# Waiting for an expert's weights block by block, and a third rounding remainder moved to GpSimd

## What is computed

```
x -> attention of 512 tokens and 32 state rows per (batch, head), 8 x 8 heads        -> 4352 rows of 512
idx = argmax(logits);  h = max(x[mask] @ w1[e], 0);  out[mask] = gate * (h @ w2[e])  -> 8 experts, 512 -> 1024 -> 512
h = x @ w_in;  g = max(h, 0) + alpha * min(h, 0);  out = g @ w_out                   -> 512 -> 2048 -> 512
```

## Time and profile before

| | us |
|---|---|
| device time, median of 3 (lowest, highest) | 1403.92 (1402.19, 1405.24) |
| device time of the profiled execution | 1405.78 |
| its span, first to last instruction | 1404.0 |
| TensorE busy in it | 1343.3 (96%) |
| VectorE, ScalarE, GpSimd busy | 826.7, 424.1, 189.4 |
| mean granted TensorE clock | 0.979 of full |

### The profile page before, as it was taken

How to read it: one execution, slowest core, us unless ns; L and a number is a source line. 1 busy time by engine, 2 the same in 40 slices (tenths; PEclk the granted TensorE clock), 3 DMA queues, 4 the chain that set the end, 5 groups by cost and what they waited for, 6 DMA issues and landing times.

```text
span 1404.0 us, 22418 instructions
## 1 busy us (share of the span) xinstructions
PE 1343.3 (96%) x7807; PEld 1159.1 (83%) x7808; DVE 826.7 (59%) x1070; ACT 424.1 (30%) x623; POOL 189.4 (13%) x234
## 2 busy tenths in 40 slices
PE   8999589999979999997899999999999999999998
PEld 7877468888868888885899999999978888888886
DVE  4777653223555435255677767778876566566653
ACT  5888241111433323144112202122322222222221
POOL 4564112211222222222000000000000000000000
PEclk9999799999999999999899999999999999999999
DMA  7785263111547433451633344333444444444453
GB/s 286 266 272 187 68 217 105 37 45 63 199 157 244 149 115 128 167 161 59 212 134 120 127 143 142 128 135 111 163 121 114 120 120 128 118 112 112 112 120 53
DMA packets 180849, 195.50 MB, mean 139 GB/s; under 512 B 25296, under 2 KB 130768, under 8 KB 180176
## 3 DMA queue, kind: packets, MB, share of 16 engines
q1 hardware_dynamic: 173552, 174.61, 39.4%
q0 software_dynamic: 6112, 19.93, 4.1%
q10 hardware_dynamic: 1152, 0.56, 0.2%
HBM read 127.16 MB, written 67.37 MB: 139 GB/s over the span
## 4 chain that ended last, share of the span: by engine, by line
PE 92%; DVE 3%; ACT 2%; issue 1%; ACTq 0%; DMA 0%; DVEq 0%; POOL 0%; POOLq 0%
PE ps_p L364 13%; PE ps_p L366 13%; PE ps_p L365 13%; PE ps_y L364 5%; PE ps_y L366 5%; PE ps_y L365 5%; PE ps_h L364 5%; PE ps_h L366 5%; PE ps_h L365 5%; PE ps_o L364 5%; PE ps_o L366 5%; PE ps_o L365 5%; PE ps_hT L1514 2%; PE ps_sr L1392 1%; PE ps_xT L1508 1%
## 5 line engine op out<-in xcount | busy, mean ns | idle before, releaser
L364 PE MATMUL ps_p<-b_hi,w_hi 128*128 128x272 f32 x896 | 259.5, 290 | 3.7 <-DVE b_lo L1227 3.7
L366 PE MATMUL ps_p<-b_hi,w_lo 128*128 128x272 f32 x896 | 259.7, 290 | 0.0
L365 PE MATMUL ps_p<-b_lo,w_hi 128*128 128x272 f32 x896 | 259.6, 290 | 0.0
L364 PEld LDWEIGHTS ps_p<-b_hi,w_hi 128*128 128x128 f32 x896 | 169.8, 190 | 4.6 <-DVE b_lo L1227 4.6
L366 PEld LDWEIGHTS ps_p<-b_hi,w_lo 128*128 128x128 f32 x896 | 170.0, 190 | 0.0
L365 PEld LDWEIGHTS ps_p<-b_lo,w_hi 128*128 128x128 f32 x896 | 169.3, 189 | 0.0
L364 PE MATMUL ps_h<-w_hi,xgT_hi 128*128 128x512 f32 x296 | 122.4, 413 | 9.7 <-DVE w_lo L952 7.7
L1147 DVE COPY hid<-ps_h 128x512 f32<-128x512 f32 x74 | 51.1, 691 | 135.2 <-PE ps_h L366 128.7
L364 PE MATMUL ps_y<-w_hi,hidT_hi 128*128 128x512 f32 x296 | 122.7, 414 | 0.0
L1149 DVE SCALAR_TENSOR_TENSOR hidT_lo<-ps_hT,hidT_hi 128x512 fp32r<-128x512 f32 x74 | 51.2, 691 | 121.2 <-ACT hidT_hi L828 121.2
L828 ACT ACTIVATE hidT_hi<-ps_hT 128x512 fp32r<-128x512 f32 x74 | 44.2, 598 | 245.1 <-PE ps_hT L1514 245.1
(11 more groups left out here) (223 smaller groups left out, 2417.7 us busy)
## 6 DMA issues: line engine op xcount, KB each, us to landing
acts<-gb SPq DMA_DIRECT2D x128, 272.0 KB, 2.1
stage<-in_moe_w SPq DMA_DIRECT2D x32, 1024.0 KB, 5.2
gt<-acts SPq DMA_DIRECT2D x32, 1024.0 KB, 6.1
xs_all<-in_xT SPq DMA_DIRECT2D x8, 1024.0 KB, 6.3
xN_all<-in_xN SPq DMA_DIRECT2D x8, 1024.0 KB, 6.2
rows_x<-xrow SPq DMA_DIRECT2D x32, 256.0 KB, 2.7
out_rows<-orow SPq DMA_DIRECT2D x32, 256.0 KB, 2.0
yz<-rows_y SPq DMA_DIRECT2D x30, 256.0 KB, 3.1
```

The lines of the kernel that those rows point to most:

```text
L364: pe.matmul(out, s_hi, m_hi, start=start, stop=False)
L365: pe.matmul(out, s_hi, m_lo, start=False, stop=False)
L366: return pe.matmul(out, s_lo, m_hi, start=False, stop=stop)
```

## The change

It has four parts.

1. TensorE waits for chunk 0 at an expert's start, and in every slot for chunk 1 before the third k block of `hidden(0)`, for chunk 2 before `result(0)`, and for chunk 3 before `result(1)`. These three waits compare with a value held in a register and stand in the slot's loop, so that they are run 37 times.
2. The low part of the third late block is made by GpSimd, after its last scatter, with a semaphore of its own, `late_lo_ready`. TensorE's P3 waits for that, and VectorE waits for it before the first write over `late_w` (`low` of P7).
3. ScalarE issues its four loads of y after two late roundings and makes the third behind them.
4. A pad of 32 columns moves `late_w`, so that it lies under the low parts of P7 and later alone.

```diff
@@ memory
+        sb("late_pad", [P, 32], c=sc)
         late_w = [t[:].rearrange("p a k f -> p (a k f)") for t in (raw_w, sum_w)] + [sb("late_w", [P, CW], c=sc)[:]]
@@ gpsimd, after the loop of slots
+            pool.wait_ge(w_hi_ready, (E + 1) * CH + 3)
+            pool.tensor_tensor(w_lo[1][:, 2 * CW:3 * CW], late_w[2], w_hi[1][:, 2 * CW:3 * CW].bitcast(F32), ALU.subtract)\
+                .then_inc(late_lo_ready, 1)
@@ scalar
+            def round_late(i):
+                act.activation(w_hi[1][:, i * CW:(i + 1) * CW], late_w[i], ACT.Copy).then_inc(w_hi_ready, 1)
+
             act.wait_ge(late_loaded, 48)
-            for i in range(3):
-                act.activation(w_hi[1][:, i * CW:(i + 1) * CW], late_w[i], ACT.Copy).then_inc(w_hi_ready, 1)
+            round_late(0)
+            round_late(1)
...
                 act.dma_start(yz[i * Q:(i + 1) * Q, S // Q, :],
                               rows_y[XT * P:XT * P + NS, i * P:(i + 1) * P]).then_inc(y_loaded, 16)
+            round_late(2)
@@ vector
-            for i in range(3):
+            for i in range(2):
                 dve.wait_ge(w_hi_ready, (E + 1) * CH + i + 1)
...
             sums_34(0)
+            dve.wait_ge(late_lo_ready, 1)
             for product in (P7, P4, P5, P3):
@@ tensor
-            def slot(s, buf):
+            def chunk_ready(e, i):
+                pe.wait_ge(w_lo_ready, CH * e + i + 1)
+
+            def slot(s, e, buf):
                 pe.wait_ge(xT_lo_ready, s + 1)
-                hidden(0, range(KD), buf).then_inc(h_ready, 1)
+                hidden(0, range(0, 2), buf)
+                chunk_ready(e, 1)
+                hidden(0, range(2, KD), buf).then_inc(h_ready, 1)
...
                 pe.wait_ge(hT_lo_ready, 2 * s + 1)
+                chunk_ready(e, 2)
                 result(0, range(0, 1), buf)
...
                 pe.wait_ge(hT_lo_ready, 2 * s + 2)
+                chunk_ready(e, 3)
                 result(1, range(KF // 2), buf).then_inc(y_ready, 1)
...
-                    pe.wait_ge(w_lo_ready, CH * e + CH)
+                    chunk_ready(e, 0)
...
-                    pe.wait_ge(w_lo_ready, E * CH + SLOT[p] + 1)
+                    if p == P3:
+                        pe.wait_ge(late_lo_ready, 1)
+                    else:
+                        pe.wait_ge(w_lo_ready, E * CH + SLOT[p] + 1)
```

More of the change, by code:

```diff
@@ L318, in build @@
         yrow_ready = sem("yrow_ready")
-        late_loaded = sem("late_loaded")
+        late_loaded, late_lo_ready = sem("late_loaded"), sem("late_lo_ready")
         raw_loaded, s1_made, sums_made, sums_stored = sem("raw_loaded"), sem("s1_made"), sem("sums_made"), sem("sums_stored")
@@ L1551, in _ @@
                     start, end = [pe.value_load(table[0:1, k, bass.ds(e, 1)], min_val=0, max_val=SLOTS) for k in (0, 3)]
-                    pe.wait_ge(w_lo_ready, CH * e + CH)
+                    chunk_ready(e, 0)
                     with upto(pe, start, end) as s:
-                        slot(s, par)
+                        slot(s, e, par)
                     pe.matmul(ps_h[0][:, 0:P], ident[:], ident[:], start=True, stop=True).then_inc(expert_done, 1)
```

## The result

The changed kernel runs in 1407.76 us (median of 22; 1403.0 to 1409.55), the kernel before, beside it on the same chip, in 1404.32 (22; 1400.13 to 1406.67). The ratio is 1.0017 [1.0009, 1.0025]: **slower by 0.17%, 1.3 to 3.5 us**. The forecast was 1403.0 with 1400.6 to 1406.2; the time lies above the range. The profiled execution took 1408.09, its span 1406.3.

A forecast was written before the change was run, and what follows sets the result against it. TensorE, busy 96% of the span, was taken as the bound, so only its stops could win. 1.1 us won at the expert's start less 0.2 lost at the entry gave 0.9 off 1403.92: 1403.0 us, range 1400.6 to 1406.2.

The forecast's parts named there:

- What bounds, and the six other starts: TensorE, busy 96% of the span, bounds the kernel; the other six expert starts do not wait and stay so.
- The turning can start at about 420.4: Fourth expert's start: VectorE's copy directly follows the four sums, so the turning starts at 420.4, not 423.71; 3.3 us sooner.
- The clock is back 4.4 us after the restart, which costs 2.2: Behind the 5.2 us stop before the turning: half clock for 4.4 us costs 2.2 of 3.3, leaving 1.1 us won.
- The price of the waits: I take 0: Three added waits and three register instructions per slot, 37 times, were taken to cost nothing.
- the rival's 0.10: Register step before `result(0)` delays the product; each slot loses 0.10 us, 3.7 in all, giving 1406.7; chance 0.12.
- the 0.09 us taken as free: Before `result(0)` in each slot: 0.09 us of cover was taken to hide the added register step.
- 0.2 lost: Last stage's entry: GpSimd's remainder holds VectorE's low parts; 0 to 0.4 us lost, 0.2 taken.
- the two readings of y: ScalarE's first load stood behind its third rounding, y there at 668.1; or behind SP's four loads, y at 669.8.
- that rival: Last stage's entry: GpSimd holds the turning of y too; low parts 2.5 us later, 1405.3; chance 0.08.
- VectorE isn't held: Last stage's entry: VectorE runs freely beside GpSimd, so the entry wins up to 2.1 us, 1400.7; chance 0.07.
- The stop simply moves whole: Expert's start: the stop moves from weights to copy, 0 won in part 1, 0.2 lost, 1404.1; inside the main case, 0.53.
- The chance for slower: Above 1406.7 or so: half the slot-price rival, a little of the turning-of-y rival, and spread; chance 0.12.

The follow-up runs named there:

- hoist: The changed kernel with VectorE's table reads for the odd expert moved ahead of the sums; 1403.73 us, ratio 1.0003 to the kernel before.
- two: The kernel before, with TensorE waiting at an expert's start for chunks 0 and 1 only, table reads not moved; 1406.74 us, ratio 1.0005.
- after: The changed kernel with all four parts, against the kernel before; 1407.76 us, ratio 1.0017.
- w_only: The kernel before with only part 1 of the change, the waits by chunk; 1407.65 us, ratio 1.0018.
- w_redundant: The kernel before with the three in-slot waits added, never holding because the expert's start still waits for all four chunks; 1404.76 us, ratio 1.001.
- w_red2: The kernel before with one extra, never holding wait per slot, before `result(0)`; 1404.49 us, ratio 0.9996.
- w_red1: The kernel before with one extra, never holding wait per slot, before the third k block of `hidden(0)`; 1404.46 us, ratio 0.9995.
- w_red3: The kernel before with one extra, never holding wait per slot, before `result(1)`; 1405.88 us, ratio 0.9994.
- e_half: The kernel before with parts 2 to 4, but GpSimd makes only 1024 of the third late block's 2048 columns, VectorE the rest; 1404.9 us, ratio 0.9998.
- two_hoist: The kernel before, starts waiting for chunks 0 and 1 only, the odd expert's table reads moved ahead of the sums; 1400.75 us, ratio 0.9977.
- two_hoist_acopy: two_hoist with ScalarE instead of VectorE copying the first half of `hid`, with its own semaphore; 1399.21 us, ratio 0.996 to the kernel before.

## Why the prediction was wrong

**What bounds, and the six other starts.** Right: TensorE is busy as long as before (1343.5), and of the six other starts behind the first none has a stop in the changed kernel.

**"The turning can start at about 420.4", 3.3 us sooner.** This step failed. The premise was that the copy is the next instruction of VectorE behind the sums. It is in the list of engine instructions, but not in the sequencer's: four table reads stand between, 2.5 us with VectorE idle. In the trace of before they ran from 419.0 to 421.8 and were hidden, because the copy came 2.92 us later anyway, waiting for TensorE; that gap was read as a wait for TensorE alone. From the end of the third expert the turning comes at 13.48 us instead of 14.32: 0.8 won, not 3.3. hoist and two show the cause: with the reads moved 11.47 and 11.48, without 13.48 and 13.47. The forecast was 11.0 on this scale (420.4 less 409.39), so with the reads out of the way it is met but for the 0.50 us of them that find no cover.

**"The clock is back 4.4 us after the restart, which costs 2.2".** The fall, its place behind the turning and the direction were right, the term too small: 5.9 us instead of 4.4, 2.7 lost instead of 2.2. What the prediction had no number for is how little the same half clock had cost before. There the slow products run while VectorE's reads keep it from the copy until about 422.1 anyway (3.19 us from the last sum's start, as in the changed kernel); the copy came at 422.53. The turning then came 14.32 us after the third expert's end, against the 13.48 that VectorE alone allows. So half clock had cost at most 0.8 us, and that is all that the change won there. In the seven kernels that stop before `ps_h` for all four chunks, 0 us of half clock lie behind the turning. In all kernels that stop over 4 us before `ps_hT` (after, w_only, hoist, two) 3.9 to 5.9 us lie behind it, and the way from the turning to the end is 1.7 to 2.7 us longer, beyond the 0.8 that the waits behind it add in w_redundant. In each of the four that is 0.15 to 0.3 us less than half of the half clock. So the same stop moved behind 18 products is dearer by its clock. These are profiles of one execution each.

**"The price of the waits: I take 0".** 0.035 us per slot, 1.3 us in 37 slots: between the 0 taken and the rival's 0.10, and at the place that the rival named, `result(0)`; w_red2 alone has it, w_red1 and w_red3 don't. The sentence with the Trainium skill's 50 to 100 ns for reading a semaphore ("Advanced Engine Details and Errata", section "Network/Comms") gave up to 0.01 beyond the cover; the run gives 0.035, and the measurement decides. The distance from `hidT_lo` to the first product, by which the prediction meant to show it, grew only where the low part is late (0.15 to 0.25 at 403); in the slot at 649 of the earlier trace rows it stayed at 0.24. Yet the ordinary slots did get longer. So the 0.09 us taken as free covered a step of 0.10 only in part, some 0.065 of it by these numbers (an estimate). The slot's length was the better test.

**The sum.** From the first slot to the third expert's end 0.7 lost (slots), then 0.8 won to the turning, then 3.5 lost to the experts' end (236.20 against 232.72), of which 0.8 are the waits and 2.7 the clock; at the entry 0.2 won. That is 3.2 us lost in the profiles; the medians differ by 3.4, and the ratio says 1.3 to 3.5. The prediction had 0.9 won. Of the 4.1 us between them the table reads make 2.5, the waits 1.5 and the clock 0.5; the entry was 0.4 better than forecast.

**The entry: "0.2 lost".** 0.2 won: GpSimd and VectorE excluded each other as the prediction had it, the size was off by 0.4, and neither of the two readings of y came. GpSimd and VectorE in the changed kernel:

```profile
669.87 6.23 POOL L691 TENSOR_TENSOR w_lo<-late_w,w_hi 128x2048 fp32r<-128x2048 f32 x1 [2.58 <-ACT w_hi L868]
```

```profile
669.36 2.28 DVE L1210 TENSOR_TENSOR w_lo<-sum_w,w_hi 128x2048 fp32r<-128x2048 f32 x1
672.63 2.50 DVE L1218 STREAM_TRANSPOSE yT<-yz 128x1152 f32<-128x1152 f32 x2 [0.99 <-DMA yz<-rows_y]
675.06 2.25 DVE L1236 TENSOR_TENSOR b_lo<-yT,b_hi 128x544 fp32r<-128x544 f32 x2
```

GpSimd was held until VectorE's block ended at 671.64, and then took 4.46 us, to 676.10 (4.56 forecast; e_half's half, from 667.00 to 669.24, took 2.24). The turning of y kept its 2.50 beside it, so that rival falls, as does "VectorE isn't held": the low parts took 2.25 instead of 1.31, 0.94 more, until GpSimd had ended. By the rule of the Trainium skill ("SBUF — State Buffer", section "Who interferes with whom"), the trace agrees: the two exclude each other whole. e_half agrees with its sentence on the order, too: GpSimd had started first and was let through first.

y itself lay between the two readings. ScalarE's first load no longer hung (0.40 us instead of 2.94), as in the first reading, and its last was issued until 667.31, 2.7 us sooner (2.19 us ahead of the idle products' start, not 0.51 behind it). But SP, which waits for all of y, went on at 672.62, 5.3 us behind the last issue and not 3.3. That is 3.12 us after the idle products' start against 3.84 before, 0.7 sooner. VectorE was free when y came, which gives 0.4 more, so the turning started 1.1 us sooner; waiting for GpSimd took 0.94 of that back.

**"The stop simply moves whole"** was named, called "half that case" and priced at 0.2 lost, inside the main case. It was the case that came, 0.8 us better at the turning and 2.7 worse behind it; its price left out that the clock comes with the stop. The rival with the slots' price was right in place and a third in size. The chance for slower took each alone; both came together, and that makes the 0.17%.

## What to carry to other kernels

Before a wait is moved, list what the waiting engine's sequencer does between two instructions, too: an idle time put down to another engine may cover register loads that will be the next bound. Where an engine works in order, one early wait on the last thing that is needed first may be all: two_hoist changes one number and moves four reads, and beats hoist, the version with three more waits (0.9977 against 1.0003, intervals apart). And look at what stands behind a stop: half clock is cheap where the work behind it is waiting for something else anyway, and dear where it is not.

## What the runs showed that was not expected

- A read of a table value by VectorE's sequencer takes 0.30 us, with its register work about 0.7; four hold the engine for 2.5 us (`DVEq` at L360, and the 2.50 ahead of the copy).
- The half clock around one and the same stop of 7.7 us ended anywhere from 10.9 to 13.7 us after the third expert's end in the seven kernels with that stop. The runs of the changed kernel cluster near 1403.1, 1405.4 and 1407.8 us, and their mean granted clock goes with it: 0.984 in the four fastest of the 22, 0.977 to 0.980 in all 15 from 1407.5 up. In the kernel before it is 0.984 at 1400.2 and 0.978 at 1406.4. Which stop the clock differs at is not shown, since one execution of each kernel was profiled. So the 5.9 us of half clock are what one run of the largest cluster had, not every run.
- A half-sized share of work for a second engine made the entry 1.3 us longer than the undivided one (18.10 against 16.80), since VectorE had to wait for GpSimd in front of the turning of y.
- Whether the reads at the other pairs' starts, or of ScalarE (stops at 399 and 468 in two_hoist_acopy), could be moved as well was not tried.
